# Zeros of the padding rows stored ahead of the turn between two layers, and one cast moved on ScalarE, in a kernel of attention and two expert layers

## What is computed

```python
def _moe_ref(x, w_in, w_out):          # x 4608x512, w_in 512x2048
    h = x @ w_in
    g = h * (1.0 / (1.0 + np.exp(-1.702 * h)))
    return g @ w_out

def _moe2_ref(x, w_gate, w_output_gate, w1, w2):   # 8 experts, 512x1024 and 1024x512
    e_idx = np.argmax(x @ w_gate, axis=1)
    gate_w = softmax(x @ w_gate)[np.arange(N), e_idx]
    eom = 1.0 / (1.0 + np.exp(-(x @ w_output_gate)))
    for e in range(E):
        mask = e_idx == e
        h = np.maximum(x[mask] @ w1[e], 0.0)
        out[mask] = gate_w[mask, None] * eom[mask, e, None] * (h @ w2[e])
    return out
```

## Time and profile before

| | us |
|---|---|
| median of 3 runs | 1329.37 |
| profiled execution | 1328.66 |
| its span, first to last instruction | 1327.0 |
| TensorE busy in it | 1306.9 |
| DVE, GpSimd, ScalarE busy in it | 624.0, 564.8, 389.5 |
| mean granted clock of TensorE | 0.998 of full speed |

### The profile page before, as it was taken

One profiled execution on the slowest core, in us unless ns is written; L12 is line 12 of the kernel. 1 busy time (PEld: TensorE's weight loads), 2 busy tenths in 40 slices (PEclk: granted clock), 3 DMA queues, 4 the chain that ended last, 5 costly groups with the idle time before them and its releaser, 6 DMA issues.

```text
span 1327.0 us, 23583 instructions
## 1 busy us (share of the span) xinstructions
PE 1306.9 (98%) x6876; PEld 1052.2 (79%) x6877; DVE 624.0 (47%) x1281; ACT 389.5 (29%) x722; POOL 564.8 (43%) x666
## 2 busy tenths in 40 slices
PE   7999999999999999999999999999999999999998
PEld 4557888888888888888888888887888888888886
DVE  4884333533433435334344343347655555555553
ACT  4773222222322222223222222233222222222221
POOL 2778944433433543344334343412343342433332
PEclk9999999999999999999999999999999999999999
DMA  9999466565465554654655546647873789548882
GB/s 383 406 391 323 150 203 192 187 180 186 165 194 182 189 176 159 179 192 155 193 182 171 177 175 176 196 162 234 245 227 100 217 247 251 164 134 261 240 246 76
DMA packets 154507, 274.20 MB, mean 207 GB/s; under 512 B 17427, under 2 KB 54676, under 8 KB 152148
## 3 DMA queue, kind: packets, MB, share of 16 engines
q1 hardware_dynamic: 97764, 203.21, 44.8%
q10 hardware_dynamic: 43728, 38.55, 11.9%
q0 software_dynamic: 12960, 31.72, 7.5%
HBM read 144.92 MB, written 100.45 MB: 185 GB/s over the span
## 4 chain that ended last, share of the span: by engine, by line
PE 93%; DMA 4%; DVE 1%; ACT 1%; issue 0%; POOL 0%; ACTq 0%; SPq 0%; POOLq 0%; DVEq 0%
PE ps L808 29%; PE ps L776 29%; PE ps L849 16%; PE ps L878 16%; DMA kvm<-in_kv 3%; PE ps L818 1%; PE ps L695 1%; DMA phT<-in_phi 0%; PE ps L676 0%; PE ps L744 0%; PE ps L668 0%; ACTq L1113 0%; POOL sc L1677 0%; ACT aT L958 0%; PE ps L709 0%
## 5 line engine op out<-in xcount | busy, mean ns | idle before, releaser
L776 PE MATMUL ps<-xs,W 128*128 (+1 forms) x1728 | 417.7, 390 | 0.9 <-DVE gate L1306 0.9
L808 PE MATMUL ps<-W,gs 128*128 128x512 f32 x1728 | 414.8, 389 | 0.1
L776 PEld LDWEIGHTS ps<-xs,W 128*128 128x128 f32 x1728 | 322.9, 188 | 70.6 <-issue 2.7
L808 PEld LDWEIGHTS ps<-W,gs 128*128 128x128 f32 x1728 | 324.3, 188 | 67.7 <-DVE gs L1311 0.5
L1306 DVE TENSOR_TENSOR gate<-ps,gate 128x512 f32<-128x512 f32 x144 | 99.6, 692 | 361.7 <-ACT gate L1048 361.4
L1048 ACT ACTIVATE gate<-ps 128x512 f32<-128x512 f32 x144 | 86.2, 598 | 462.3 <-PE ps L776 444.8
L1736 POOL CAST whi<-raw 128x512 fp32r<-128x512 f32 x128 | 84.5, 660 | 321.6 <-DMA raw<-in_moe_w 321.6
L878 PE MATMUL ps<-W,chT 128*128 (+1 forms) x936 | 218.1, 389 | 1.4 <-DVE chT L1473 1.4
L849 PE MATMUL ps<-W,cx 128*128 (+1 forms) x936 | 218.8, 390 | 0.3 <-issue 0.3
L878 PEld LDWEIGHTS ps<-W,chT 128*128 128x128 f32 x936 | 175.6, 188 | 38.3 <-issue 1.8
L849 PEld LDWEIGHTS ps<-W,cx 128*128 128x128 f32 x936 | 175.4, 188 | 37.2 <-issue 0.9
(11 more groups left out here) (163 smaller groups left out, 783.1 us busy)
## 6 DMA issues: line engine op xcount, KB each, us to landing
W<-expert_scratch SPq DMA_DIRECT2D x24, 2048.0 KB, 11.2
raw<-in_moe_w SPq DMA_DIRECT2D x128, 256.0 KB, 2.8
expert_scratch<-whi SPq DMA_DIRECT2D x128, 256.0 KB, 2.7
expert_scratch<-raw SPq DMA_DIRECT2D x128, 256.0 KB, 3.0
cq<-ch ACTq DMA_DIRECT2D x156, 128.0 KB
kvm<-in_kv SPq DMA_DIRECT2D x15, 1152.0 KB, 12.6
crec<-record_scratch POOLq DMA_DIRECT2D x160, 64.0 KB
qT<-in_q SPq DMA_DIRECT2D x16, 576.0 KB, 12.1
```

Source lines behind the costliest of these rows:

```text
L776: mm = pe.matmul(ps[:, f % 2, :], W[:, col:col + P], xs[:, bass.ds(x0 + (x_lo * K1 + c) * T, T)], start=(c == 0 and w_lo + x_lo == 0), sto ...
L808: mm = pe.matmul(ps[:, 2 + s, :], gs[:, f % 2, g_lo, s * P:(s + 1) * P], w_out_sb[:, f, w_lo, :], start=(f == 0 and g_lo + w_lo == 0), sto ...
```

## The change

It has three parts.

1. `pad` stores only the 12 meta words of its 128 rows (48 B a row).
2. A new `fill`, issued by SyncE for each expert behind its wait for `b_first` and ahead of its wait for mm1 step 8, stores the 512 x columns of 9 x 128 rows, from the end of each region at that time (a copy of `base`, which then holds tiles 0 to 6, that DVE makes with the first expert). GpSimd waits for all eight, in the last tile, ahead of the scatters of tile 7.
3. On ScalarE the two casts of block 1 (`act_h_hi(1, 1)`) stand ahead of the four moves of block 2.

```diff
@@ pad, and the new fill
             end = eng.value_load(tbl[0:1, 7, e:e + 1], min_val=e * REGION, max_val=e * REGION + N)
-            eng.dma_start(rec_dram[bass.ds(end, P), :], padrec[:]).then_inc(b_pad, 16)
+            eng.dma_start(rec_dram[bass.ds(end, P), DM:REC], padrec[:, DM:REC]).then_inc(b_pad, 16)
+
+        OPEN = 2 * SUB + 1
+
+        def fill(eng, e):
+
+            end = eng.value_load(tbl[0:1, 7, NE + e:NE + e + 1], min_val=e * REGION, max_val=e * REGION + N - 2 * T)
+            eng.dma_start(rec_dram[bass.ds(end, OPEN * P), 0:DM].rearrange("(j p) d -> p j d", p=P),
+                          padrec[:, 0:DM].rearrange("p (o d) -> p o d", o=1).broadcast_to([P, OPEN, DM])).then_inc(b_fill, 16)
@@ SyncE
             first_e = sp.value_load(tbl[0:1, 6, 0:1], min_val=0, max_val=NE - 1)
+            for e in range(NE):
+                fill(sp, e)
             sp.wait_ge(b_h, (NT - 1) * C1 + C1 // 2)
@@ ScalarE
+            act_h_hi(1, 1)
             act_h_move(2, 0)
-            act_h_hi(1, 1)
@@ DVE, first_expert
+                step(dve.tensor_copy(tbl[0:1, 7, NE:2 * NE], base[0:1, SUB, :]), False)
@@ GpSimd
+                    if i == 4 and last:
+                        pool.wait_ge(b_fill, 16 * NE)
                     if i == 4 and not first:
                         scatter_records(t - 1)
```

More of the change, by code:

```diff
@@ L306, in build @@
         b_fs = sem("first_expert_steps")
+        b_fill = sem("padding_zeros_stored")
         b_end = sem("record_ends")
```

## The result

The changed kernel takes **1364.22 us** (median of 4 runs, 1363.19 to 1366.47); before, measured beside it, 1329.02 us. The ratio is 1.0266, 95% interval 1.0253 to 1.0278: slower by 35 us. The profiled execution took 1363.19 us, its span is 1361.6 us, mean granted clock 0.986.

The account below looks back on a forecast made before the run. TensorE, busy 98% of the span, was taken to bound the kernel. W wait +30.6, clock +1.7 and turn -1.2 gave +31.1 us on the profiled 1328.66; with the median 0.7 higher, forecast 1360.5 us, range 1347 to 1384.

Parts of the forecast that it names:

- The wait for W: Before TensorE's first expert product: W chunks 0 and 1 queue behind the fill, start moves from 891.91 to 922.5, +30.6 us.
- the clock: TensorE behind the new stall: granted clock falls mostly to 1.2 GHz for a while, +1.7 us, ends 0 and 4.
- the turn: Last tile's expert blocks up to block 3: small pads and earlier cast shorten TensorE's gaps, -1.2 us, ends -1.7 and +1.3.
- The fill: SyncE's queue in the last tile: 18.87 MB starts at 853.2 us, drains at 387 GB/s, lands at 906.3 us.
- the rival of half the rate: Fill stores drain at 204 GB/s, 92.5 us: +43.7 us, 1404 us; chance 0.07.
- The HBM side is a lower ceiling: Strided fill stores drain at only 352 GB/s: 1365.3 us; chance 0.17.
- The queue does not hold W back: Engines share fill and W loads; W is in time, GpSimd's wait before tile 7's scatters decides: 1361.9 us; chance 0.09.
- The fill is hidden: Fill fits into SyncE's 22.1 us wait, only the turn is left: 1328.2 us, not slower; chance 0.05.
- Covered, by 1.8 us only: Before block_y(0): W chunks 2 and 3 are there at 940.3 us, block_y(0) needs them at 942.1 at the earliest.
- Bytes and issue time in the old rows go together: Reason for taking the low end of the small pads' cost; at full old cost TensorE waits up to 1.0 us more.
- Pads issued in under 4 us: Sign expected in the trace: SyncE issues the eight small pads in under 4 us, where the old ones took 11.30.
- The swap: ScalarE's cast ahead of block 2's moves: the 1.43 us gap closes, but moves start 2.3 us later, delaying block_y(2).

Follow-up runs that it names:

- w_first: Changed kernel with the fill issued behind the loads of W chunks 0 and 1 instead of ahead of them: 1372.54 us, ratio 1.0325.
- open5: Changed kernel with a fill of 5 blocks of 128 rows for each expert in place of 9: 1342.50 us, ratio 1.0098.
- old_pads: Changed kernel with pads of whole rows again, the fill kept: 1365.51 us, ratio 1.0267.
- no_chunk_waits: Changed kernel, but SyncE does not wait for one W chunk of the first expert before issuing the next: 1357.30 us, ratio 1.0207.
- ncw_again: Second measurement of the changed kernel without SyncE's waits between the first expert's W chunks: 1356.76 us.
- static_no_cast: Changed kernel without fill, GpSimd's wait for it, or swap; small pads stay, zeros these inputs need stored in the first tile: 1327.47 us, ratio 0.9984.
- warm: Changed kernel with 34 products of zeros on TensorE between the last mm2 and the first expert product: 1364.32 us, ratio 1.0265.
- cast_only: Kernel before with only the cast of block 1 put ahead of block 2's moves: 1329.33 us against 1329.65, ratio 0.9998.
- static: Changed kernel without fill and GpSimd's wait for it; small pads and swap stay, zeros these inputs need stored in the first tile: 1327.85 us, ratio 0.9986.
- no_cast: Changed kernel with the swap undone, block 2's moves ahead of block 1's cast: 1363.89 us, ratio 1.0256.
- warm_no_chunk_waits: Changed kernel without SyncE's waits between the first expert's W chunks, plus 32 products of zeros in TensorE's wait: 1357.11 us, ratio 1.0206.

## Why the prediction was right, and where it was not

**The sum.** Forecast 1360.5 in 1347 to 1384, measured 1364.2. Against the profiled execution's own time: +31.1 forecast, +34.5 measured (1363.19 less 1328.66). The wait for W and the clock came as forecast within 0.2 us each; the 3.5 us that are missing are in the turn.

**The fill.** Its place (853.2, measured 852.7), its rate (387, measured 378 GB/s) and its end (scatters released at 906.3, measured 907.25) held. That the first expert product came at 922.34 us, forecast 922.5, is in part luck: chunk 0 landed at 911.8 us, 1.3 earlier than forecast, and chunk 1 took 10.3 us instead of 9.2. The rule of the Trainium skill (DMA: Bandwidth & Descriptors, Specifications), an HBM limit of about 358 GB/s for one core, is not borne out: the fill held 378 GB/s for 46 us. What the prediction did not have was that the fill's issues would block SyncE, 36.52 us for eight. It cost nothing, as the W loads could not have moved before anyway. In its range, the longest store of 2880 KB is 2.95 MB and not 2.88: as a whole 209 GB/s, and the rival of half the rate at 1402 us instead of 1404. Nothing hangs on it.

**The rivals.** "The HBM side is a lower ceiling" had 1365.3 us, which is nearer to the measured 1364.2 than my 1360.5. The time alone cannot tell the two apart; the trace can. At 352 GB/s the fill would have ended 4.8 us later and the first expert product come at 927.3; it came at 922.34, and the rate was 378. "The queue does not hold W back" was wrong as to which wait ends last. Its own case, the fill and W sharing the engines, was not run; w_first has W there in time by another order, and gives 1372.5 where the rival had 1361.9. Of these 10.6 us, 7.8 are the fill, which starts only behind two W loads (871.91 us) and lets the scatters go at 924.75 instead of 917; most of the rest is in the chain behind, 12.5 us from there to the transposes where 10 were forecast. So this wait is about as large as the rival said. "The fill is hidden" fell with the result, and open5 shows that even 5 blocks of 9 cost 13 us.

**TensorE's clock.** Forecast +1.7, measured +1.9 by the first product (4.80 for 2.88 us). The size is luck in part: up to the second expert product, the traces that waited for W and whose clock fell lost 1.5 (old_pads) to 2.9 us (open5), and two traces of one kernel 1.8 and 2.8 (no_chunk_waits, ncw_again). One reading was weak too: the row of 908 to 919 us ends 0.5 us behind the 1.43 us gap and could hardly show a fall; that there was none is shown by block_y's 48 matmuls behind it, 11.15 us, as in static_no_cast (11.14). But warm shows that it was not a term of its own: with the clock kept, the time is the same. The term was sized rightly and put on the path wrongly; it lay beside a DMA wait that the prediction did not have.

**The turn.** This is the step that failed: "I take **-1.2 us**, ends -1.7 and +1.3". In the changed kernel it was +2.3 (34.69 less 30.43 and 1.92). The working took the turn of before and shifted it as a block. But the shift put it beside other DMA traffic. Before, chunk 3 was issued at about 894.9 and block 0's moves at 900.4; now chunk 3 is issued at 930.8 and the moves at 932.7, so the moves share the engines with 2.1 MB and, from 938.6 on, with the scatters of tile 8. They land at 942.7, DVE waits 4.16 us for them, block_y(0) 2.02 us, and the clock falls a second time (0.67), so that two block_y take 12.79 us where they took 11.15. The prediction asked of chunks 2 and 3 only whether block_y(0) would find them there ("Covered, by 1.8 us only"), not what they would do to the moves. Chunk 3 did land in time, at 941.9 us (940.3 forecast); it was the moves that came late, and block_y(0) began at 946.00 where the terms of the sum give 943.8 (922.5 + 1.7 + 19.56). no_chunk_waits takes 4.3 us out of this stretch and so shows the cause. With chunk 3 out of the way, and the slow first product counted apart, the turn is 1.8 us shorter than before: what the prediction said of the gaps was right, and what it left out was larger.

**The pads.** "Bytes and issue time in the old rows go together" is wrong here: 8.03 and 8.11 us for whole and small pads, and at the old place small pads save 1.3 to 2.1 us of 11. "Pads issued in under 4 us", one of the signs, did not come true. The low end was still the right choice, for a reason that the prediction also had: the row table sets block 3, not the pads. SyncE had issued the last pad by 951.1 us and then stood for DVE's table before it loaded block 3 (waits of SyncE, 940 to 965 us):

```profile
SPq L638 <- DVE small L1597: 3.9, 1, 3.9
```

The small pads' worth is the traffic that they spare the moves. static_no_cast shows it (gap 1.43 to 0.43 us, some 2 us less): there ScalarE casts block 1 at 915.86 us, 23.43 behind the first expert product, where it was 24.43 before (916.34). The Trainium skill's rule on transfers under 512 B (same page, same section) shows no cost here: a small pad of 128 rows of 48 B landed in 1.4 to 3.7 us, a whole one in 2.4 to 4.8 (old_pads).

**The swap.** Its working, that the gap moves from block 1 to block 2, is what cast_only shows. With the small pads the second gap closes too (static, 0.25 us), but the medians tell no difference between with and without.

**What stays open.** Whether no_cast is faster or slower than the changed kernel: the median says 0.3 us less, the single trace 1.5 us more in span. Whether the small pads without any zeros of x would do for all inputs was not tried; the rows would hold what the memory held before. And what an earlier fill would cost, issued from 812 us on, is open.

## What to carry to other kernels

A store placed "in the last tile" starts when its queue gets there, not when its data are ready: read the issuing engine's timeline first, then divide the bytes by the rate of the nearest saturated row; here these two numbers, with the two loads queued behind the stores, gave the loss of 30 us before anything ran. When a stall shifts a stretch, work that stretch out again beside the transfers that it now meets, instead of moving it as a block. And a cost that lies beside another wait (here the clock) is not a term of the sum until that wait is gone.

## What the runs showed of the hardware

- Issuing large stores blocked SyncE: eight of 2.36 MB took 36.52 us to issue (18.24 us for stores of 1.31 MB), the first 0.43 us and the longest 4.96. They drained more slowly still, 6.2 us each at 378 GB/s, and a store landed 20.3 us (median) after the start of its issue.
- 378 GB/s was held for 46 us by stores of 2048 B rows, 2096 B apart.
- The granted clock fell behind a wait of 2.02 us (0.67 at 945 to 950 us) and behind one of 2.62 us (first product 4.59 us), but not behind the waits of 1.16 (warm), 1.43 (before) and 1.49 us (warm_no_chunk_waits). Behind the 8.76 us of open5 it was still 0.50 from 901 to 906 us.
- The start of SyncE's late DMAs moved by 3.5 us between two executions of one kernel (854.37 us in no_chunk_waits, 850.88 in ncw_again), and with the fill it went into the time (3.4 us of span). Without the fill TensorE's own work covers it: the first W load went out at 854.41 us in cast_only and at 852.98 in static, and neither waits for W.
